# Gated stage on one core: the rank matmuls between the two products of block six, the turns and logits inside the next tile's x product

## The reference

```python
a = x @ w1                                    # [2304, 1024]
b = x @ w2
x = (a * b @ w3) @ w_out                      # [2304, 512]
...
logits = x @ w_gate                           # [2304, 8]
noise_scale = np.log1p(np.exp(x @ w_noise))
noisy_logits = logits + noise_scale * noise
top2 = np.argpartition(-noisy_logits, 2, axis=1)[:, :2]
...
h = np.maximum(x[mask] @ w1[e], 0.0)
out[mask] += top2_w[mask, k, None] * (h @ w2[e])
```

## Time and profile before

| | |
|---|---|
| median of 3 runs | 1150.83 us (1149.87 to 1151.39) |
| profiled execution | 1149.4 us, span 1147.5 us |
| TensorE busy, share of the span | 1078.7 us (94%) |
| VectorE | 473.9 us (41%) |
| ScalarE | 371.3 us (32%) |
| GpSimd | 541.9 us (47%) |
| mean granted clock of TensorE | 0.977 of full speed |
| gated stage, first to last x product | 313 to 642 us of the span |

### The profile page before, as it was taken

The page is one execution under the profiler, slowest core; times in us unless marked ns, Lnnn a source line. Parts: engine busy times, 40 slices in busy tenths (PEclk is TensorE's granted clock), DMA queues, the critical chain, the costliest instruction groups (busy, mean ns, idle before and its releaser), DMA issues. The chain is left out here.

```text
span 1147.5 us, 18575 instructions
## 1 busy us (share of the span) xinstructions
PE 1078.7 (94%) x6320; PEld 975.5 (85%) x6321; DVE 473.9 (41%) x1073; ACT 371.3 (32%) x898; POOL 541.9 (47%) x368
## 2 busy tenths in 40 slices
PE   4999999998999999999999549999999999999997
PEld 3888888887798989899999449898989898989895
DVE  5887877866512424241414442222222222222221
ACT  3777777765411213231313142121212121212110
POOL 7776777740000020201111133786878787877752
PEclk9999999998999999999999759999999999999999
DMA  8644444426397010101000063535353535353303
GB/s 230 149 100 92 94 93 101 103 52 195 91 368 278 2 55 0 55 9 46 21 35 34 30 231 128 114 97 144 100 143 117 121 115 123 110 128 119 46 1 46
DMA packets 69638, 118.11 MB, mean 103 GB/s; under 512 B 7776, under 2 KB 25312, under 8 KB 69600
## 3 DMA queue, kind: packets, MB, share of 16 engines
q1 hardware_dynamic: 60960, 97.61, 28.8%
q0 software_dynamic: 8640, 20.00, 8.8%
HBM read 81.00 MB, written 36.59 MB: 102 GB/s over the span
## 5 line engine op out<-in xcount | busy, mean ns | idle before, releaser
L782 POOL DMA_INDIRECT expert_rows<-x_rows,slot_idx x36 | 40.1, 1113 | 311.9 <-DVE slot_idx L925 302.8
L1387 PE MATMUL ps_hT<-xT_high,ew_high 128*128 128x256 f32 (+3 forms) x512 | 156.8, 306 | 1.9 <-DVE xT_low L1473 1.9
L1387 PE MATMUL ps_hT<-xT_low,ew_high 128*128 128x256 f32 (+3 forms) x512 | 155.7, 304 | 0.0
L1387 PE MATMUL ps_hT<-xT_high,ew_low 128*128 128x256 f32 (+3 forms) x512 | 155.2, 303 | 0.0
L1404 PE MATMUL ps_y<-ew_high,hT_high 128*128 128x512 f32 x320 | 129.3, 404 | 1.4 <-DVE hT_low L1480 1.4
L1404 PE MATMUL ps_y<-ew_low,hT_high 128*128 128x512 f32 x320 | 126.9, 397 | 0.0
L1404 PE MATMUL ps_y<-ew_high,hT_low 128*128 128x512 f32 x320 | 126.9, 396 | 0.0
L1480 DVE SCALAR_TENSOR_TENSOR hT_low<-ps_hT,hT_high 128x384 fp32r<-128x384 f32 (+1 forms) x128 | 62.9, 492 | 152.2 <-ACT hT_high L1442 152.2
L1442 ACT ACTIVATE hT_high<-ps_hT 128x384 fp32r<-128x384 f32 (+1 forms) x128 | 56.0, 438 | 156.7 <-PE ps_hT L1387 156.2
L1277 POOL DMA_INDIRECT out<-y_tile,out_rows x40 | 63.1, 1577 | 90.1 <-DVE y_tile L1489 85.8
L1489 DVE TENSOR_SCALAR y_tile<-ps_y,weight_of 128x512 f32<-128x512 f32 x40 | 30.0, 751 | 179.0 <-PE ps_y L1404 179.0
(11 more groups left out here) (198 smaller groups left out, 2683.4 us busy)
## 6 DMA issues: line engine op xcount, KB each, us to landing
spare<-e_w SPq DMA_DIRECT2D x16, 1024.0 KB, 5.3
w_raw<-e_w SPq DMA_DIRECT2D x16, 1024.0 KB, 8.3
q_raw<-qT SPq DMA_DIRECT2D x36, 288.0 KB, 4.3
k_raw<-kT SPq DMA_DIRECT2D x36, 288.0 KB, 5.5
expert_rows<-zeros SPq DMA_DIRECT2D x8, 1290.0 KB, 14.3
ex_rows<-expert_rows SPq DMA_DIRECT2D x40, 258.0 KB, 3.9
out<-zeros SPq DMA_DIRECT2D x11, 512.0 KB, 10.8
v_raw<-v SPq DMA_DIRECT2D x16, 256.0 KB, 4.9
```

The source lines that it names most:

```text
L782: nc.gpsimd.indirect_dma_start(out=rows_dram, out_offset=bass.IndirectOffsetOnAxis(ap=slot_idx[:, k, t:t + 1], axis=0), in_=x_rows[:, t, : ...
L1387: mm = nc.tensor.matmul(ps_hT[q % HS][:, 0:rows.stop - rows.start], lhsT[:, c, f * P:(f + 1) * P], rhs[:, c, rows], start=(n == 0), stop=( ...
```

## The change

Only TensorE's order in the gated stage changes. The same instructions are issued.

- The rank of group g - 1 no longer stands behind block 5 of group g, but inside block 6, between its product into `ps_a` and the one into `ps_b`.
- The turn of tile t - 1 no longer stands behind x product t, but inside it, behind its first nine matmuls (f = 0, 1, 2).
- The logit of tile t - 1 stands inside the same x product, behind 18 matmuls (f = 5). Before, the logit of tile 0 stood behind x product 2, and that of tile 1 behind block 0 of the next group (for the last group, behind everything).
- Turn and logit of tile 2 stay behind blocks 0 and 1 of the next group, or at the end.

```diff
                     for ps, hi, lo in ((ps_a, w1_high, w1_low), (ps_b, w2_high, w2_low)):
+                        if f == 6 and ps is ps_b and not first:
+                            rank(g - 1)
                         n = 0
...
                     mm.then_inc(ab_done, 1)
                     if f == 0 and not first:
-
-                        logit(g - 1, TT - 2, False)
                         turn(g - 1, TT - 1, False)
                     if f == 1 and not first:
                         logit(g - 1, TT - 1, False)
-                    if f == 5 and not first:
-                        rank(g - 1)
                 for t in range(TT):
...
                             n += 1
+                        if t and f == 2:
+                            turn(g, t - 1, first)
+                        if t and f == 5:
+                            logit(g, t - 1, first)
                     mm.then_inc(x_done, 1)
-                    if t:
-                        if t > 1:
-                            logit(g, t - 2, first)
-                        turn(g, t - 1, first)
 
             groups(pe, emit)
-            logit(GROUPS - 1, TT - 2, False)
             turn(GROUPS - 1, TT - 1, False)
```

## The result

The changed kernel takes 1167.68 us (median of 5 runs, 1165.77 to 1170.86) against 1150.83 before. The ratio is 1.0153, with a 95% interval of 1.0137 to 1.0168: slower by 17 us. The forecast was 1173.3 in a range of 1162 to 1178, and slower. The profiled execution took 1166.6 us, its span is 1164.7, 17.2 more than before.

What follows compares the result with a forecast made beforehand. TensorE was taken to bound the gated stage, busy 323.1 of 328 us. Waiting and restart terms summed to +12.0 us, clock falls added +10.5: +22.5, giving 1173.3 us against 1150.8, own range 1170 to 1176.5, 8-in-10 range 1162 to 1178.

Steps and rivals of the forecast that it cites:

- rival 1: Stalls at full clock: the new waits at the turn of tile 0 occur but TensorE's speed stays up, 1162.8 us; chance 0.17.
- ranks: Block 6: twelve matmuls ahead of the rank cover its wait for `r_both` in the five looped groups, -4.9 us.
- stall, groups 1 to 4: x product 1: TensorE waits at the turn of tile 0 for ScalarE's copy, 3.42 to 3.53 us each, +13.65 us.
- more restarts, groups 0 to 4: x products: turns and logits interrupt the matmul streams more, +0.12 us a group, +0.6 us over five (0 to 1.2).
- last group and tail, without clock: Group 5: with a 2.76 us wait at the turn of tile 0, last logits copied at 650.15 against 647.48, +2.67 us.
- clock: TensorE's clock falls to 0.50 behind each of the five new stalls in x product 1, 2.1 us each, +10.5 us.
- Rival 2: Transfers land before the turn of tile 0 comes up in x product 1, so no wait: 1146.4 us, faster; chance 0.05.
- Rival 3: TensorE stays longer at low clock behind each of five stalls, 3.5 us each: 1180.3 us; chance 0.08.

## Why the prediction was right, and where its terms were off

The direction, the mechanism and its place were right: `x_taken` of tile 0 comes with the landing of all six transfers, and the turn moved in front of it. The time lay in the range, 5.6 us under the forecast. That it did is owed to the wide range, which reached down to rival 1; the forecast's own, 1170 to 1176.5, was missed. Term by term, from the profiled executions:

| term | forecast | measured |
|---|---|---|
| ranks | -4.9 | -6.4 |
| stall, groups 1 to 4 | +13.65 | +13.4 |
| more restarts, groups 0 to 4 | +0.6 | +1.3 |
| last group and tail, without clock | +2.67 | +2.8 |
| clock | +10.5 | +5.6 |
| sum | +22.5 | +16.7, of 17.1 at the last logits |

The measured ranks are the 277.01 less 270.64 of the run with the ranks alone. The restarts are read from two runs without stalls, which both have the ranks in block 6 and the tile semaphores and differ only in the place of turns and logits. From the first to the last x product 0, first with these inside the x products, then where they were before:

```profile
349.47 0.39 PE L1027 MATMUL ps_x<-wo_high,ab_high 128*128 128x512 f32 x1
...
621.04 0.39 PE L1027 MATMUL ps_x<-wo_high,ab_high 128*128 128x512 f32 x1
...
347.94 0.39 PE L1029 MATMUL ps_x<-wo_high,ab_high 128*128 128x512 f32 x1
...
618.22 0.39 PE L1029 MATMUL ps_x<-wo_high,ab_high 128*128 128x512 f32 x1
```

271.57 against 270.28, that is 1.3, a little over the forecast's range of 0 to 1.2. The stall is the profile's idle time and 0.17 for each, 13.8, less the 0.4 by which the run with the ranks alone is longer than the 270.28 (its turns still wait a little for their copies). The clock is what a group takes beyond 54.31, the length with turns and logits inside and no stall, and beyond its own stall: 60.33 less 54.31 and 3.42 is 2.6, and 59.29 less 54.31 and 3.41 is 1.6. In the last group it is 1.4: 26.74 us from its x product 0 to the logits, against 22.57 in the run without the stall and 2.77 of stall. Of the 0.4 that is left over, 0.3 arises before the first x product 0 (348.24 against 347.95), and 0.1 is not placed.

- **The clock** is the term that failed: +5.6 in place of +10.5. The forecast read from two rows that an idle time near 3 us loses the clock, and took five falls of 2.1. Three of five fell in the profile, and the longest of the five, 3.37, did not. The size of one was nearly right (1.4, 1.6 and 2.6 against the 2.1 taken), so most of the miss is the two falls that did not come. Rival 1 (no fall at all) and the forecast each held for some of the groups, and the kernel lies between them. The sentence from the Trainium skill, "TensorE: Matmul & The Clock Gate", Part 4, that transposes don't count in the way that matmuls do, was not decided: in the last group the stall of 2.60 lost the clock in the changed kernel, and one of 2.65 with the same turn behind it kept it in the run with the turns alone. A turn stands behind every one of the new stalls, so no run here tells the two cases apart.
- **The ranks** were undersized because I priced the wait by the idle column. That column begins where the modelled end of the last matmul is. But a matmul that starts at 393.06 lets the next one start at 393.23, and the rank came at 394.37: 1.14 from start to start, not 0.97. For the new stall I had reckoned from start to start, and there the number was exact. In the middle of block 6 the rank also costs less, 0.62 to the second matmul behind it (395.28 to 395.90) against 0.73 behind an idle time (394.37 to 395.10). Together that is 1.25 of the 1.27 seen.
- **The tail** of this pair of profiles gained nothing from what was taken out of it: 22.57 us with the turns inside and no stall, 22.52 before. But 22.52 is the shortest of the five profiles with the old tail; the others have 22.99, 23.55, 23.95 and 24.13, since the clock falls earlier in them. So the shorter tail may well save up to 1 us on the mean, which the forecast had at 0.1, and the comparison with one profile of before hides it.
- Rival 2 (faster, 1146.4) is what the run with the tile semaphores made true, at 1144.6. Rival 3, 3.5 us for each fall, did not occur in the changed kernel, whose longest fall cost 2.6; one fall of the run with the turns alone came near it with 3.2.

## What to carry to other kernels

Before a consumer is moved earlier, look at how late its input is, and not at whether anyone waits for it now: a wait of another engine that costs nothing (here ScalarE's for the transfers) becomes TensorE's as soon as its consumer moves in front of it. Reckon a stall from start to start, and look for the next wait behind the moved instruction too. Where one semaphore counts several transfers and the consumer needs only some of them, issuing them part by part with a semaphore for each part removes the wait, and moving work around it can be spared.

## What the runs showed of the hardware

Whether the clock falls behind a stall is not settled by its length over a wide range. Counted over the waits for copies and ranks within the six groups, in the profiles of before, after and these runs (idle time as the profile lists it):

| idle, us | stalls | clock fell |
|---|---|---|
| 4.0 to 4.8 | 5 | 5 |
| 2.6 to 3.4 | 10 | 6 |
| 1.2 to 2.0 | 5 | 3 |
| 0.5 to 1.0 | 14 | 0 |

No count here sets 1.9 us apart from 4.8; only the stalls of 1 us and less are clearly another case. Even one and the same idle time can go either way. The first matmul of the stage, left out of the table, stands behind 2.8 us of idle in all twelve profiles. The clock fell behind it in ten, and the changed kernel among them. It was kept in the run with the turn behind 15 matmuls, shown here, and in one of the two profiles of the ranks with tile semaphores, the other of which lost it:

```profile
314.14 0.44 PE L1009 MATMUL ps_a<-x_high,w_high 128*128 128x384 f32 x1 [2.80 <-DVE x_low L953]
...
311.00:318.00 7.00, 4.20 (x24) 1.00 0.46 101
```

What decides between the two no run shows. The table leaves out the tail as well. There TensorE works in pieces of 1 to 2 us, with idle times of 0.7 to 0.8 between them, and in all twelve profiles the clock had fallen within 5 us of the start of the last turn. So short idle times spared the clock within the groups, and not there.

Each fall costs 1.4 to 3.2 us here. One might expect that a kernel with such stalls spreads more from run to run. The runs don't show that: the changed kernel's five lie 5.1 us apart, but the runs of the kernel before, which waits no longer than 1 us at a time within its groups, lie 4.5 to 5.6 apart in sets of 11 to 17.
